# First layer of a fused attention and two-MLP kernel by seven block products, with v transposed on VectorE and most norms moved

## The reference, cut to what matters

```python
N, C = 6016, 256
qn = q / (norm(q, axis=1) + 1e-6);  kn = k / (norm(k, axis=1) + 1e-6)
a = softmax(kn.T @ qn / tau)                      # 256 x 256, over channels
x = (v @ a)                                       # 6016 x 256
h = x @ w_in                                      # 256 -> 2048
g = where(h >= 1, h, where(h <= -1, 0, (h + 1)**2 / 4))
x = g @ w_out                                     # 2048 -> 256
xn = x / sqrt(mean(x * x, axis=-1) + 1e-6) * rms_g
gate = xn @ w_gate                                # 256 -> 1536
out = (gate * sigmoid(gate) * (xn @ w_val)) @ w_out2
```

## Time and profile before

| | |
|---|---|
| median of 3 runs | 1176.92 us (1176.17 to 1176.92) |
| the profiled execution | 1175.06 us, its span 1173.1 us |
| TensorE busy | 1150.8 us, 5918 matmuls |
| weight loads, VectorE, ScalarE busy | 985.9, 864.0, 626.0 us |
| front, up to the first produce | about 0 to 65 us |
| phase 1, phase 2 | about 65 to 597 us, 597 to 1173 us |

### The profile page before, as it was taken

How to read it: one execution, slowest core, us unless ns; L and a number is a source line. 1 busy time by engine, 2 the same in 40 slices (tenths; PEclk the granted TensorE clock), 3 DMA queues, 4 the chain that set the end, 5 groups by cost and what they waited for, 6 DMA issues and landing times.

```text
span 1173.1 us, 15842 instructions
## 1 busy us (share of the span) xinstructions
PE 1150.8 (98%) x5918; PEld 985.9 (84%) x5918; DVE 864.0 (74%) x1367; ACT 626.0 (53%) x1041; POOL 1.0 (0%) x9
## 2 busy tenths in 40 slices
PE   8999999999999999999988999999999999999998
PEld 7868888888888888888977888888888888888997
DVE  6568788788888898898877876666667666667555
ACT  5444554554444545546556655556446446545554
POOL 0000000000000000000000000000000000000000
PEclk9999999999999999999999999999999999999999
DMA  9700010010100110100031002002002001000100
GB/s 345 255 1 18 18 37 29 26 55 18 37 18 19 37 36 19 50 19 1 19 108 55 14 1 73 1 1 72 1 1 73 1 1 51 18 1 1 37 1 32
DMA packets 34894, 46.88 MB, mean 40 GB/s; under 512 B 2050, under 2 KB 25346, under 8 KB 34818
## 3 DMA queue, kind: packets, MB, share of 16 engines
q1 hardware_dynamic: 34818, 45.88, 11.6%
HBM read 33.56 MB, written 12.32 MB: 39 GB/s over the span
## 4 chain that ended last, share of the span: by engine, by line
PE 92%; DVE 3%; ACT 2%; issue 1%; DMA 1%; SPq 0%; DVEq 0%; ACTq 0%
PE ps L953 14%; PE ps L955 14%; PE ps L954 14%; PE ps L1050 10%; PE ps L1051 9%; PE ps L1052 9%; PE ps L1077 5%; PE ps L1075 5%; PE ps L1079 5%; PE ps L1090 3%; PE ps L974 1%; PE ps L966 1%; DVE cv L733 1%; DMA qk_sb<-in_k_dram 1%; ACT out_sb L370 1%
## 5 line engine op out<-in xcount | busy, mean ns | idle before, releaser
L387 ACT ACTIVATE act_sb<-ps 128x512 f32<-128x512 f32 (+1 forms) x192 | 113.0, 588 | 219.2 <-PE ps L955 219.0
L1050 PE MATMUL ps<-xc_hi,wc_hi 128*128 128x512 f32 (+1 forms) x504 | 203.3, 403 | 12.9 <-DVE cv L733 5.9
L1051 PE MATMUL ps<-xc_lo,wc_hi 128*128 128x512 f32 (+1 forms) x504 | 197.1, 391 | 0.0
L1052 PE MATMUL ps<-xc_hi,wc_lo 128*128 128x512 f32 (+1 forms) x504 | 196.3, 390 | 0.0
L634 DVE SCALAR_TENSOR_TENSOR act_sb<-act_sb 128x512 f32<-128x512 f32 (+1 forms) x192 | 130.3, 678 | 69.8 <-ACT act_sb L387 68.1
L1079 PE MATMUL ps<-wo_hi,h_lo 128*128 128x256 f32 x564 | 159.1, 282 | 0.0
L1077 PE MATMUL ps<-wo_lo,h_hi 128*128 128x256 f32 x564 | 159.1, 282 | 0.0
L1075 PE MATMUL ps<-wo_hi,h_hi 128*128 128x256 f32 x564 | 158.9, 282 | 0.0
L953 PE MATMUL ps<-v_hi,w_hi 128*128 128x512 f32 (+1 forms) x384 | 150.0, 391 | 0.0
L953 PE MATMUL ps<-g_hi,wo_hi 128*128 128x512 f32 (+1 forms) x384 | 148.0, 386 | 1.0 <-DVE g_lo L641 1.0
L955 PE MATMUL ps<-g_hi,wo_lo 128*128 128x512 f32 (+1 forms) x384 | 147.9, 385 | 0.0
(11 more groups left out here) (104 smaller groups left out, 1717.1 us busy)
## 6 DMA issues: line engine op xcount, KB each, us to landing
v_raw<-in_v_dram SPq DMA_DIRECT2D x11, 512.0 KB, 3.8
x_scratch<-y_sb SPq DMA_DIRECT2D x11, 512.0 KB, 3.4
out_dram<-out_sb SPq DMA_DIRECT2D x11, 512.0 KB, 3.0
qk_sb<-in_q_dram SPq DMA_DIRECT2D x10, 512.0 KB, 11.0
qk_sb<-in_k_dram SPq DMA_DIRECT2D x10, 512.0 KB, 12.6
xraw<-x_scratch SPq DMA_DIRECT2D x10, 512.0 KB, 4.7
w_in_raw<-in_moe_w_in_dram SPq DMA_DIRECT2D x4, 512.0 KB, 11.7
wo_raw<-in_moe_w_out_dram SPq DMA_DIRECT2D x4, 512.0 KB, 10.7
```

The source lines that it names most:

```text
L1050: nc.tensor.matmul(dst, w_h, x_h, start=fresh, stop=False, skip_group_check=True)
L1051: nc.tensor.matmul(dst, w_h, x_l, start=False, stop=False, skip_group_check=True)
L1052: nc.tensor.matmul(dst, w_l, x_h, start=False, stop=True, skip_group_check=True).then_inc(made[p], 1)
```

## The change

Phase 1 now has the form of phase 2: tiles of 1024 tokens (6, the last 896) and 8 pair groups n1 in each; a group is 2x2 blocks (token halves, two hidden blocks) by seven products of three matmuls, and the output product of group n1-1 lies between them as 8 pieces of three 512-column matmuls. `make_w1` is followed by `w1_copy`, `w1_sums`, `w1_high`, `w1_low` per pair. v is loaded so that VectorE's 32x32 block transposes (`transpose_v`) give a whole transpose; only the first tile goes through TensorE, during the scores. The activation is max(h, (0.5 clip(h, -1, 1) + 0.5)^2), by a clip on VectorE, a square on ScalarE and a maximum on VectorE, on 1024 columns at a time (early: cells 0 and 1; late: 2 and 3). y is stored raw; the norms of the first four half tiles are made in phase 1 from a reloaded copy, the other eight in phase 2 inside xraw. In the diff, lines of "..." stand for what is left out.

```diff
-PIECES = {"p6": 2, "p4": 3, "p5": 3}
+PIECES1 = {"p6": 1, "p4": 3, "p5": 4}
+PIECES2 = {"p6": 2, "p4": 3, "p5": 3}
...
 # SyncE
+            def load_v(T):
+                n = half(T)
+                for h in range(2):
+                    tok = token(T, h)
+                    for a in range(CT):
+                        for g in range(4):
+                            c = a * P + 32 * g
+                            sp.dma_start(vstage[32 * g:32 * g + 32, h, a, 0:n].rearrange("p (b c) -> p b c", c=32),
+                                         v[0, tok:tok + n, c:c + 32].rearrange("(b p) c -> p b c", p=32)
+                                         ).then_inc(vstage_loaded, 16)
...
+            for T in range(WT):
+                if T:
+                    store_y(T - 1, 0)
+                    store_y(T - 1, 1)
+                if 1 <= T <= JOBS:
+                    load_y(T - 1)
+                if T + 2 < WT:
+                    sp.wait_ge(vT_ready, 4 * (T + 1))
+                    load_v(T + 2)
+                if 1 <= T <= JOBS:
+                    store_x(T - 1)
...
 # ScalarE, phase 1
+            for n1 in range(N1):
...
+                if n1:
+                    c12_copy(n1 - 1)
+                if p == 0 and T:
+                    xc_high(T, "p3")
+                spare(s1, "p1", c11_ready, n1, n, n1 % 2, s1_ready)
+                if n1:
+                    square(n1 - 1, 1)
+                spare(s7, "p7", c22_ready, n1, n, 3, s7_ready)
+                spare(s2, "p6", c21_ready, n1, n, n1 % 2, s2_ready)
...
+                if p == 1 and T:
+                    copy_y(T - 1, 1)
+                if n1:
+                    g_high(n1 - 1, 1)
...
+                square(n1, 0)
+                if p == 0 and T:
+                    copy_y(T - 1, 0)
+                if 1 <= T <= JOBS:
+                    if p == 2:
+                        y_squares(T - 1)
+                    if p == 3:
+                        y_squares_high(T - 1)
+                    if p == 4:
+                        root_mean_square(T - 1)
+                    if p == 5:
+                        spread_rows(T - 1)
+                if T == WT - 1:
+                    if p in (2, 4, 6):
+                        wc_high(p // 2 - 1)
+                    if p in (4, 6):
+                        wo2_high(p // 2 - 2)
...
+                g_high(n1, 0)
...
 # ScalarE, phase 2, second half of a pair
                 h_high(r, 0, 0)
...
+                if job is not None:
+                    if j in (0, 2):
+                        y_squares(job + j // 2)
+                        y_squares_high(job + j // 2)
+                    if j in (1, 3):
+                        root_mean_square(job + j // 2)
+                        spread_rows(job + j // 2)
                 if not into:
                     h_high(r, 1, 0)
...
 # VectorE, phase 1
+            def clip(n1, late):
...
+                nc.vector.tensor_scalar(q_sb[:, rows, 0:n], h_sb[n1 % 2][:, rows, 0:n], -1.0, 1.0, ALU.max,
+                                        ALU.min).then_inc(clip_ready, 1)
...
+                if n1:
+                    clip(n1 - 1, 1)
+                if p == 0 and T:
+                    xc_low(T, "p4")
+                if n1:
+                    g_low(n1 - 1, 0)
+                combine(h[:, 0, 0:n], s1, s1_ready, "p2", n1, n, 2, c11_ready)
+                if n1:
+                    maximum(n1 - 1, 1)
+                if p == 0 and T:
+                    xc_low(T, "p5")
+                combine(h[:, 1, 0:n], s2, s2_ready, "p4", n1, n, 3, c21_ready)
+                clip(n1, 0)
+                if n1:
+                    g_low(n1 - 1, 1)
...
+                combine(h[:, 2, 0:n], s7, s7_ready, "p5", n1, n, B, c22_ready)
+                if p == 0 and T:
+                    xc_low(T, "p3")
+                if 1 <= T <= JOBS and p == 4:
+                    transpose_sums(T - 1)
+                maximum(n1, 0)
...
 # VectorE, phase 2, second half of a pair
                 multiply11(r)
...
+                if job is not None and j in (0, 2):
+                    y_squares_sum(job + j // 2)
                 if not into:
                     h_low(r, 0, 0)
                 combine21(cv, r, 1)
...
                     multiply2(r, 0)
+                if job is not None and j in (0, 2):
+                    y_squares_low(job + j // 2)
+                if job is not None and j in (1, 3):
+                    correct_rms(job + j // 2)
                 combine22(cv, r, 1)
+                if job is not None and j in (1, 3):
+                    transpose_rows(job + j // 2)
...
 # TensorE, phase 1
+            for n1 in range(N1):
...
+                for name in ORDER:
...
+                    product(name, n1, w1c_hi[p][:, ws, :], w1c_lo[p][:, ws, :], half(T))
+                    if n1 == 0 and name in ("p4", "p5"):
+                        make_w1(2 if name == "p4" else 3)
+                    if n1:
+                        for i in range(done, done + PIECES1.get(name, 0)):
+                            piece1(n1 - 1, i)
+                        done += PIECES1.get(name, 0)
+                    if 1 <= T <= JOBS and p == 4 and name == "p5":
+                        sum_squares(T - 1, n1)
```

More of the change, by code:

```diff
@@ L546, in _ @@
+            for r in range(N2):
+                T, j = divmod(r, PAIRS2)
+                n, G, X = half(T), N1 + 2 * r, WT + T
+                into, onto = j == PAIRS2 - 1 and T + 1 < WT, j == 0 and T > 0
+                job = 4 + 2 * (T - 1) if 1 <= T < WT - 1 else None
                 if onto:
-                    xc_high(T, "p5")
-                    xc_high(T, "p3")
+                    xc_high(X, "p5")
+                    xc_high(X, "p3")
                     h_high(r - 1, 1, 0)
@@ L563, in _ @@
                 if r == 0:
-                    wc_high(2)
-                    wo2_high(0)
-                if r == 2:
-                    spread_rows(TILES - 1)
+                    g_high(N1 - 1, 1)
+                if r == 1:
+                    copy_y(WT - 1, 1)
                 act.wait_ge(c11_ready, G + 1)
@@ L782, in _ @@
                                             ALU.add).then_inc(added, 1)
+                if c in (8, 9):
+                    for i in ((0, 1) if c == 8 else (2, 3)):
+                        xc_sum(0, i)
+                for p in {10: ORDER[0:3], 11: ORDER[3:5], 12: ORDER[5:7]}.get(c, []):
+                    xc_low(0, p)
             steps = [0]
@@ L864, in _ @@
+            for r in range(N2):
+                T, j = divmod(r, PAIRS2)
+                X = WT + T
+                into, onto = j == PAIRS2 - 1 and T + 1 < WT, j == 0 and T > 0
+                more = T + 1 < WT
+                job = 4 + 2 * (T - 1) if 1 <= T < WT - 1 else None
                 if onto:
-                    xc_low(T, "p6")
+                    xc_low(X, "p6")
                     multiply2(r - 1, 0)
                     multiply2(r - 1, 1)
-                    xc_low(T, "p4")
+                    xc_low(X, "p4")
@@ L912, in _ @@
-                if r == 3:
-                    wc_sums(5)
-                if more and 2 <= j <= 4 and T:
-                    xc_sum(T + 1, j - 2)
-                if r == 4:
-                    for i in range(3):
-                        xc_sum(1, i)
+                    wc_low(2, 0)
+                    wc_low(2, 1)
+                if r in (1, 2, 3):
+                    wc_sums({1: 3, 2: 4, 3: 5}[r])
+                if job is not None and j in (1, 3):
+                    transpose_sums(job + j // 2)
@@ L1072, in piece @@
                 first = (1 if late else 0) == f
-                start, stop = j == 0 and first and c % 2 == 0, j == PAIRS - 1 and not first
+                start, stop = j == 0 and first and c % 2 == 0, j == PAIRS2 - 1 and not first
                 u = 2 * j + f
@@ L1174 @@
+            r = N2 - 1
+            for i in range(2 * chunks(WT - 1)):
+                piece2(r, i)
 _INS = ["q", "k", "v", "tau", "moe_w_in", "moe_w_out", "moe2_w_gate", "moe2_w_val", "moe2_w_out", "moe2_rms_g"]
```

1197 lines of the change are left out of this document (599 added, 598 removed).

## The result

| | kernel before | changed kernel |
|---|---|---|
| median of the runs | 1176.66 us | 1230.03 us |
| lowest to highest | 1176.17 to 1176.92 | 1228.78 to 1234.05 |
| profiled execution | 1175.06 us, span 1173.1 | 1234.05 us, span 1232.3 |
| first long Silu of phase 2 starts at | 610.34 us | 632.35 us |
| from there to the end of the span | 562.8 us | 599.9 us |

The ratio is 1.046, with a 95% interval from 1.0435 to 1.0485: slower by 53 us, as forecast in sign, and inside the range. The forecast, 1213, is 17 us short of it, and 21 us short of the profiled execution, the slowest of the four. Of the 59 us between the two profiled spans, 22 were lost before phase 2 and 37 in it.

The account below looks back on a forecast made before the run. TensorE, busy 98% of the span, was taken as the only bound. Against 1175.06 us: -41.4 for matmuls and transposes removed, +11+6.4+13.8+11.3+9+3+24.8 for waits, sum +37.9, so 1213 us; range 1170 to 1245.

Parts of the forecast that it names:

- Products, -32.0: First layer's product on TensorE: 192 units of 6 matmuls become 48 groups of 21, 256 to 224 us.
- Ring stall, +11: Phase 1's wait loop through ScalarE and VectorE, late copy to g_low: TensorE stalls 0.25 us per group, 45 groups.
- Tile boundary, 1.3 each: Phase 1, group 0 of tiles 1 to 5: xc_low and copy_y delay the ring, +6.4 us in all.
- Norm in phase 1, 3.45 per tile: Norm steps ahead of ring links in groups 4 and 5 of tiles 1 to 4, +13.8 us in all.
- Weights in the last tile, +11.3: Layer-two conversions in groups 2, 4, 6: wc_high waits for wc_sums, delaying c12_copy 2.5 us, 4.0 with wo2_high.
- First tile, +9; front, +3: First tile: w1 copied, summed, split between groups, +9 us; front: v0 loaded ahead of later q and k chunks, +3.
- Phase 2, 2.0 and 1.1 per norm pair: Phase 2's eight norms delay c22 2.0 us in steps 0 and 2, 1.1 in 1 and 3; +24.8 in all.
- every wait added on TensorE goes onto it one for one: Premise: TensorE, busy 98% of the span, is the only bound, so each added wait lengthens the time equally.
- Rival 1: Matmul count decides: delays at the late-half hand-over, ring and c22, are hidden by overlap; 1146 us, chance 0.13.
- rival 2: Ring some 0.5 to 1 us looser, so each written delay loses that; 1170 to 1190 us, chance 0.12.
- rival 3: VectorE's clip in phase 1's ring runs at single rate, 1.22 us, adding 48: 1261 us, chance 0.08.
- rival 4: The v loads, read in 128 B runs, come late: 19 us late, 1232 us, chance 0.05.

Follow-up runs that it names:

- experiment 1: Changed kernel with VectorE's g_low of the early half put ahead of the late half's clip in phase 1: 1239.77 us.
- experiment 5: Changed kernel with 12 unread 256-column matmuls filling TensorE's wait ahead of p3 in phase 2's pairs j 0 and 2, tiles 1 to 4: 1223.86 us.
- experiment 6: Changed kernel, both phases' norm work and wc_high moved: 1176.40 us; its faster kernel adds w1 work one pair per group and g_low early in some groups: 1172.40 us.

## Why the prediction was right in sign and 17 us short

- **Products, -32.0: too large by some 6 us in phase 1.** The term used 0.227 us per 512-column matmul. The new products start 0.233 us apart (fourteen starts from 202.16 to 205.19 in experiment 1, 3.03/13), and TensorE alone needs some 10.4 us for a group, not 10.2: some 9 us over 45 groups, to which the products' 21 matmuls give 21 x 0.006 = 0.13 each, or 6 us. Phase 2's pairs are slower too where both kernels issue nearly the same instructions: 15.63 against 15.46 in the middle of its first tile, 0.07 to 0.1 in the last two pairs of the others. Outside the norm pairs that comes to 1.6 us; in them it is part of the figures below. No term stood for that, and why is open.
- **Ring stall, +11: right.** 10.65 less 10.42 is 0.23, where 0.25 was forecast, and the chain runs in the order given.
- **Tile boundary, 1.3 each: 1.03** (11.68 less 10.65), 5 us in place of 6.4.
- **Norm in phase 1, 3.45 per tile: 2.6 for group 4, 1.1 for group 5** with the clock at full, 3.7, 14.8 us in place of 13.8.
- **Weights in the last tile, +11.3: 11.8** (the sum over 9.56 of the five groups behind the first), with the two peaks at 3.95 where 4.0 was forecast, and half-clock stretches about the last three groups that aren't taken out.
- **First tile, +9; front, +3.** TensorE's first make_w1 matmul starts at 63.13, at 58.04 in the kernel before: 5.1. Group 1 has 4.0 over the steady group, group 2 1.3 in some executions; the rest of the 9 I can't separate from the front.
- **Phase 2, 2.0 and 1.1 per norm pair: 2.0 to 2.65 and 1.15** at full clock, against the same pairs of the kernel before. 20.1 + 9.1 = 29 in place of 24.8. The cover for normalise held: the fifth pair of tiles 1 to 3 takes 15.77 against 15.68.
- **The step that failed: "every wait added on TensorE goes onto it one for one".** It holds for waits of some tenths. Behind 13 of 30 waits of 1.84 to 1.88 us, and behind some of the pairs of waits of 1.18 and 0.41 us in groups 5, the clock was at 0.50 for some 3 us, and 1.55 us went on top (experiment 5). The profiled execution has seven periods with it in phase 2's pairs and in groups 5 of tiles 1 to 4 (19.9 three times and 19.7; 13.3 three times), 10.9 of the 21 us by which it is over the forecast; one more is in group 2 of the first tile. It is the largest single part of that miss; the median execution, 4 us shorter, will have fewer. Three further stretches lie about the start of phase 2, where the kernel before has two of its own; what these cost isn't separated. That the result lies inside the range, with a cost of some 11 us that no term held, is in part luck.
- **Signs.** The waits stand where they were forecast: 2 us of p3 eight times (1.6 to 1.9), 4 in the last tile (3.18 for s1), 1.2 and 0.4 in groups 5. Two signs were off: the count of matmuls is down by 210, not some 300, and TensorE's busy share fell to 95%, not 92%.

Rival 1 (1146) and rival 2 fell with the ring at 10.65, which has none of the slack that they needed; rival 3 with the clip at 694 ns; rival 4 with loads that no matmul waits for. The faster kernel of experiment 6 shows how far the forecast's account reaches: with most of the delays taken out the change is worth nothing to 4 us, not the 41 of its matmuls. What stays is the ring's 0.25 per group, the boundaries, the front, slower products, and in phase 2 2.1 us per tile (96.07 against 93.95 in tile 1), 9 in all.

## What to carry to other kernels

When a change makes the bounding engine's work smaller but closes a ring of waits through the others, price the written order, not the shares: here 210 matmuls fewer became 53 us more, and the same instructions in other places took all of it back. Idle time on an engine is cover only for what has its operands by then and isn't already covering something else: two of my own edits failed on just that. A wait of TensorE of the size seen here, 1.9 us, should be priced with the chance of the slow stretch behind it, here 13 in 30 times 1.55 us, and filling it with matmuls that nobody reads can pay.

## What the runs showed of the hardware that I had not expected

- The granted clock fell to 0.50 behind single waits of 1.84 to 1.88 us, and not behind the same wait cut to 0.43 us. The same place shows it in one execution and not in the next (13.3 or 11.77 us for group 5). That this makes most of the spread of 5 us between the changed kernel's runs is not shown; it fits their mean granted clocks, 0.980 in the run of 1234.05 us and 0.984 in that of 1228.78.
- The same 512-column matmul starts 0.227 us after its predecessor in the kernel before's phase 1 and 0.233 in the new one. It isn't the form of the product: in phase 2 the three products ahead of the same two pieces start 0.2275 us apart in the kernel before (764.75 to 766.57, nine starts) and 0.234 in the changed one (724.79 to 726.66). Buffers lie elsewhere in SBUF and in PSUM; no run here tells whether that is it.
